# A routed two-layer kernel: expert slots of one size class per expert, of up to 512 tokens, in place of slots of 128 tokens

## The reference

```python
def attn(q, k, v, a):               # per batch (4) and head (8), 768 steps, 48 wide
    S = 0                           # complex 48 x 48
    for t in range(768):
        S = a[t][:, None] * S + outer(k[t], v[t])     # |a| clipped to 0.999
        y[t] = q[t] @ real(S)

def layer_a(x):                     # 3072 tokens
    logits = (x / |x|) @ (emb / |emb|).T / tau
    e = argmax(logits)
    return softmax(logits)[e] * (relu(x @ w1[e]) @ w2[e])

def layer_b(x):
    out = x
    for the tokens with x @ w_skip > 0:
        logits = x @ w_gate; e = argmax(logits)
        out = x + softmax(logits)[e] * (relu(x @ w1[e]) @ w2[e])
```

## Time and profile before

| what | us |
|---|---|
| median of 3 runs | 987.97 |
| lowest and highest | 987.32 and 994.53 |
| the profiled execution | 994.6 |
| its span in the profile | 993.0 |
| PE busy | 783.8 (79%) |
| DVE, ACT, POOL busy | 543.3, 454.0, 238.2 |

### The profile page before, as it was taken

The page is one execution under the profiler, slowest core; times in us unless marked ns, Lnnn a source line. Parts: engine busy times, 40 slices in busy tenths (PEclk is TensorE's granted clock), DMA queues, the critical chain, the costliest instruction groups (busy, mean ns, idle before and its releaser), DMA issues.

```text
span 993.0 us, 20046 instructions
## 1 busy us (share of the span) xinstructions
PE 783.8 (79%) x5035; PEld 680.6 (69%) x5036; DVE 543.3 (55%) x1395; ACT 454.0 (46%) x771; POOL 238.2 (24%) x267
## 2 busy tenths in 40 slices
PE   0598878968789896388989988898987179799991
PEld 0276757757677786277878877787877168788891
DVE  2556666767657654346555555656565226346630
ACT  6765526536436343064445444453642045344430
POOL 3307062170622411002211122222211113031120
PEclk9888688978959897599999999999999689899996
DMA  8361531815314171534222222324222216444200
GB/s 160 64 137 33 93 77 33 145 32 100 74 32 88 41 246 62 175 120 152 90 96 84 98 95 96 91 92 159 93 88 80 76 33 228 150 167 152 93 25 18
DMA packets 178428, 98.45 MB, mean 99 GB/s; under 512 B 148204, under 2 KB 167436, under 8 KB 178380
## 3 DMA queue, kind: packets, MB, share of 16 engines
q1 hardware_dynamic: 169612, 77.26, 28.7%
q0 software_dynamic: 8768, 20.64, 6.4%
HBM read 82.62 MB, written 21.85 MB: 105 GB/s over the span
## 4 chain that ended last, share of the span: by engine, by line
PE 57%; issue 16%; DVE 9%; ACT 6%; DVEq 4%; DMA 2%; ACTq 2%; SPq 1%; POOL 1%; POOLq 0%
PE bank L1510 10%; PE bank L1511 9%; PE bank L1512 9%; PE bank L1392 4%; PE bank L1381 3%; PE bank L1408 3%; PE bank L1370 3%; DVEq L1169 3%; PE bank L1409 3%; PE bank L1529 2%; PE bank L1357 2%; PE bank L1358 2%; PE bank L1354 1%; PE bank L1552 1%; PE bank L1419 1%
## 5 line engine op out<-in xcount | busy, mean ns | idle before, releaser
L1510 PE MATMUL bank<-w2h,hh 128*128 x344 | 125.7, 365 | 15.8 <-DVE w2l L1175 6.8
L1510 PE MATMUL bank<-w1h,xh 128*128 (+1 forms) x258 | 111.0, 430 | 15.2 <-DVE xl L1187 13.8
L1511 PE MATMUL bank<-w2l,hh 128*128 x344 | 121.8, 354 | 0.0
L1512 PE MATMUL bank<-w2h,hl 128*128 x344 | 121.4, 353 | 0.0
L1511 PE MATMUL bank<-w1l,xh 128*128 (+1 forms) x258 | 104.7, 406 | 0.0
L1512 PE MATMUL bank<-w1h,xl 128*128 (+1 forms) x258 | 104.5, 405 | 0.0
L831 ACT ACTIVATE hid<-bank 128x512 f32<-128x512 f32 x86 | 51.2, 598 | 107.5 <-PE bank L1512 105.9
L568 POOL DMA_INDIRECT rows_b<-yg,idx_b x27 | 26.9, 997 | 267.5 <-DVE yg L1274 267.5
L1510 PEld LDWEIGHTS bank<-w2h,hh 128*128 128x128 f32 x344 | 69.0, 201 | 22.3 <-issue 22.1
L867 ACT ACTIVATE hh<-bank 128x512 fp32r<-128x512 f32 x86 | 46.2, 589 | 71.2 <-PE bank L1529 71.0
L1305 DVE TENSOR_TENSOR hl<-bank,hh 128x512 fp32r<-128x512 f32 x86 | 55.3, 684 | 38.9 <-ACT hh L867 38.9
(11 more groups left out here) (211 smaller groups left out, 1838.6 us busy)
## 6 DMA issues: line engine op xcount, KB each, us to landing
raw<-in_moe_w SPq DMA_DIRECT2D x32, 1536.0 KB
xg<-rows_a POOLq DMA_DIRECT2D x27, 196.5 KB, 2.8
ar<-in_a_re SPq DMA_DIRECT2D x24, 192.0 KB, 3.6
...
```

The lines of the kernel that those rows point to most:

```text
L1510: t.matmul(out_, high[:, at], wh, start=c_ == 0, stop=False)
L1511: t.matmul(out_, high[:, at], wl, start=False, stop=False)
L1512: i = t.matmul(out_, low[:, at], wh, start=False, stop=c_ == n_ - 1)
```

## The change

Slots now hold up to 512 tokens of one expert (four tiles), so that an expert has one slot as long as it has no more than 512 tokens: `NS` falls from 31 to 13. A slot's length is one of 256, 320, 384, 448 or 512 columns, the smallest that holds its tokens. In the first product the weights are the stationary operand and the tokens move, which gives the hidden rows transposed, as the second product wants them; in A the second product is made in the same way, and its result (features by tokens) goes through products with the identity and gate_w at once, so that rows and B's logits come out of one set of products (`gate_w` holds the identity beside the gate columns, 137 wide). In B the second product stays as it was, tile by tile. PE has a copy of each product for each of the five lengths.

```diff
-NS = NT + E - 1
-NSP = 32
+NS = N // 512 + E - 1
+TJ = 4
+WIDE = TJ * P
+SIZES = (256, 320, 384, 448, 512)
```

```diff
+def row_out(b, c):
+    sp.wait_ge(s_y, B * c + b + 1)
+    sp.dma_start(x_a[bass.ds(b * S + c * P, P), :], ysb[:, b, :]).then_inc(s_x[b], 16)
-pool.wait_ge(s_idx, B * c + b + 1)
-g.indirect_dma_start(rows_a, bass.IndirectOffsetOnAxis(idx_a[:, b:b + 1], 0), ysb[:, b, :], None,
+pool.wait_ge(s_idx, 2 * c + b // 2 + 1)
+g.indirect_dma_start(list_of[0], bass.IndirectOffsetOnAxis(idx_a[:, b:b + 1], 0), token[:, c, b:b + 1], None,
+                     bounds_check=E * CAP - 1, oob_is_err=False).then_inc(s_put[b], 16)
...
+def members(s, par):
+    at = 0 if s == 0 else pool.value_load(tab[0:1, BASE + s:BASE + s + 1], min_val=0, max_val=E * CAP - WIDE)
+    g.dma_start(idx_g[:, par, :, 0:1 + m], list_of[m][bass.ds(at, WIDE), :].rearrange("(j p) w -> p j w", p=P),
+                allow_slow_non_contiguous=True).then_inc(s_list[m], 16)
+def gather(s, par):
+    pool.wait_ge(s_list[m], 16 * (s + 1))
+    for j in range(TJ):
+        g.indirect_dma_start(xg[:, par, j, 0:wide], None, rows, bass.IndirectOffsetOnAxis(idx_g[:, par, j, 0:1], 0),
+                             bounds_check=N - 1, oob_is_err=False).then_inc(s_xg[par][m], 16)
...
+if m == 0:
+    pool.wait_ge(s_side, s)
+else:
+    pool.wait_ge(s_yg[m], TJ * s)
+members(s + 1, par)
+pool.wait_ge(s_xT[m], KC * s)
+if m == 0:
+def scatter(s, par):
+    if m == 0:
+        pool.wait_ge(s_send, s + 1)
+        for j in range(TJ):
+            g.indirect_dma_start(list_of[1], bass.IndirectOffsetOnAxis(idx_b[:, par, j:j + 1], 0), pay[:, par, j, :], None,
+                                 bounds_check=E * CAP - 1, oob_is_err=False).then_inc(s_rows[par][m], 16)
+        pool.wait_ge(s_row, s + 1)
+    else:
+        pool.wait_ge(s_yg[m], TJ * (s + 1))
+    for j in range(TJ):
+        g.indirect_dma_start(out, bass.IndirectOffsetOnAxis(idx_o[:, par, j:j + 1], 0), yg[:, par, j, :], None,
+                             bounds_check=N - 1, oob_is_err=False).then_inc(s_rows[par][m], 16)
```

```diff
-for j in range(HP):
-    t.transpose(PY[:, j * DP:(j + 1) * DP], yT[:, b % 2, j * P:(j + 1) * P], ident[0:DP, 0:DP])
-for j in range(HP):
-    i = t.matmul(PY[:, HP * DP:HP * DP + E], yT[:, b % 2, j * P:(j + 1) * P], emb_T[:, j, :], start=j == 0, stop=j == HP - 1)
+for j in range(HP):
+    i = t.matmul(PY[:, j * DE:(j + 1) * DE], yT[:, b % 2, j * P:(j + 1) * P], aug[:, j, :], start=True, stop=True)
...
+    d.tensor_tensor(sum_a[:, :], sum_a[:, :], two_a[:, :], ALU.add).then_inc(s_sum, 1)
+dve.wait_ge(s_y, B * c + b + 2)
+d.reduce_max(mx_p[:, :], lg, AX.X).then_inc(s_mx, 1)
...
+d.tensor_tensor(oh_a[:, b:b + 2, :], each(ch_p[:, :]), pair(first_of[:, :]), ALU.is_equal).then_inc(s_oh, 1)
+d.tensor_tensor(at_f[:, :, :], PR.rearrange("p (t e) -> p t e", e=E), oh_a[:, b:b + 2, :], ALU.mult).then_inc(s_at, 1)
+d.tensor_tensor(two_a[:, :], oh_a[:, b, :], oh_a[:, b + 1, :], ALU.add).then_inc(s_two, 1)
+dve.wait_ge(s_at, k_ + 1)
+d.reduce_sum(at_s[:, :], at_f[:, :, :], AX.X).then_inc(s_at1, 1)
...
+d.tensor_scalar(idx_a[:, b:b + 2], at_s[:, :], -1.0, float(NOWHERE), ALU.mult, ALU.add).then_inc(s_idx, 1)
...
+    pe.wait_ge(s_sum, k_)
+pe.wait_ge(s_added, B * C if last else B * c + b + 3)
+two = PR.rearrange("p (t e) -> p t e", e=E)
+t.matmul(two, before_t[:, :], oh_a[:, b:b + 2, :], start=True, stop=False)
+t.matmul(two[:, 1, :], minus[:, :], oh_a[:, b, :], start=False, stop=False)
+t.matmul(two, minus[:, :], sum_a[:, :].unsqueeze(1).to_broadcast([P, 2, E]), start=False, stop=False)
+t.matmul(two, minus[:, :], starts[:, :].unsqueeze(1).to_broadcast([P, 2, E]), start=False, stop=True).then_inc(s_rank, 1)
```

In the layers the engines are written anew. ACT takes out each product and splits weights in pieces between them, DVE likewise:

```diff
+def up_out(s, size, run):
+    def parts(n):
+        for f in range(FC):
+            act.wait_ge(s_h[m], FC * s + f + 1)
+            a.activation(hh[:, f, 0:n], U[f % 3][:, 0:n], ACT.Relu).then_inc(s_hh[m], 1)
+            if f == 0:
+                act.wait_ge(s_w2in[m], run * 16)
+            high_part(w2h, raw2, HD, f).then_inc(s_w2h[m], 1)
+    sizes(size, parts)
...
+def parts(n):
+    for f in range(FC):
+        dve.wait_ge(s_hh[m], FC * s + f + 1)
+        d.scalar_tensor_tensor(out=hl[:, f, 0:n], in0=U[f % 3][:, 0:n], scalar=0.0, in1=hh[:, f, 0:n].bitcast(F32),
+                               op0=ALU.max, op1=ALU.subtract).then_inc(s_hl[m], 1)
+        dve.wait_ge(s_w2h[m], FC * s + f + 1)
+        low_part(w2l, w2h, raw2, HD, f).then_inc(s_w2l[m], 1)
+        if f == 2:
+            between()
+sizes(size, parts)
```

PE, with `n` columns of the slot, U three banks in turn, and `size` the number of tiles less 2:

```diff
+def rows_in(s, par, size):
+    pe.wait_ge(s_xg[par][m], (s - par) * 32 + 64)
+    if n_or_more(0, s, 1):
+        pe.wait_ge(s_hl[m], FC * s)
+    for tiles in (2, 3, 4):
+        with pe.If(size == tiles - 2):
+            for k_ in range(KC):
+                for j in range(tiles):
+                    i = t.transpose(U[k_][:, j * P:(j + 1) * P], xg[:, par, j, k_ * P:(k_ + 1) * P], ident[:, :])
+                i.then_inc(s_xT[m], 1)
+def up(s, n):
+    for f in range(FC):
+        if f >= 3:
+            pe.wait_ge(s_hl[m], FC * s + f - 2)
+        for k_ in range(KC):
+            wh = w1h[:, k_ * F + f * P:k_ * F + (f + 1) * P]
+            wl = w1l[:, k_ * F + f * P:k_ * F + (f + 1) * P]
+            t.matmul(U[f % 3][:, 0:n], wh, xh[:, k_, 0:n], start=k_ == 0, stop=False)
+            t.matmul(U[f % 3][:, 0:n], wl, xh[:, k_, 0:n], start=False, stop=False)
+            i = t.matmul(U[f % 3][:, 0:n], wh, xl[:, k_, 0:n], start=False, stop=k_ == KC - 1)
+        i.then_inc(s_h[m], 1)
+def down_a(s, n):
+    for d_ in range(KC):
+        if d_ == 2:
+            pe.wait_ge(s_yw, KC * s + 1)
+        for f in range(FC):
+            if d_ == 0:
+                pe.wait_ge(s_hl[m], FC * s + f + 1)
+                pe.wait_ge(s_w2l[m], FC * s + f + 1)
+            wh = w2h[:, f * HD + d_ * P:f * HD + (d_ + 1) * P]
+            wl = w2l[:, f * HD + d_ * P:f * HD + (d_ + 1) * P]
+            t.matmul(DN[d_ % 2][:, 0:n], wh, hh[:, f, 0:n], start=f == 0, stop=False)
+            t.matmul(DN[d_ % 2][:, 0:n], wl, hh[:, f, 0:n], start=False, stop=False)
+            i = t.matmul(DN[d_ % 2][:, 0:n], wh, hl[:, f, 0:n], start=False, stop=f == FC - 1)
+        i.then_inc(s_o[m], 1)
+def down_b(s, j, last):
+    if j >= 2:
+        pe.wait_ge(s_yg[m], TJ * s + j - 1)
+    elif n_or_more(0, s, 1):
+        pe.wait_ge(s_yg[m], TJ * s)
+    at = slice(j * P, (j + 1) * P)
+    for f in range(FC):
+        if j == 0:
+            pe.wait_ge(s_hl[m], FC * s + f + 1)
+            pe.wait_ge(s_w2l[m], FC * s + f + 1)
+        wh, wl = w2h[:, f * HD:(f + 1) * HD], w2l[:, f * HD:(f + 1) * HD]
+        t.matmul(DN[j % 2][:, 0:HD], hh[:, f, at], wh, start=f == 0, stop=False)
...
+with pe.If(size == tiles - 2):
+    for d_ in range(KC):
+        pe.wait_ge(s_yw, KC * s + d_ + 1)
+        for j in range(tiles):
+            if d_ == 0 and j == 3:
+                pe.wait_ge(s_yw, KC * s + 2)
+            i = t.matmul(R[j][:, d_ * GE:(d_ + 1) * GE], yw[:, d_, j * P:(j + 1) * P], gate_w[:, d_, :], start=True, stop=True)
+    i.then_inc(s_res, 1)
...
+def by_length(length, part):
+    for i, n in enumerate(SIZES):
+        with pe.If(length == i):
+            part(n)
...
+length, size = number(VAR, s, 4), number(TIL, s, 2)
+if more:
+    size_ = number(TIL, s + 1, 2)
+pe.wait_ge(s_w1l[m], s + 1)
+pe.wait_ge(s_xl[m], KC * s + KC)
+by_length(length, lambda n: up(s, n))
+if m == 0:
+    if n_or_more(0, s, 1):
+        rank_next(s - 1)
+    by_length(length, lambda n: down_a(s, n))
+else:
+    down_b(s, 0, False)
+if more:
+    with pe.If(used > s + 1):
+        rows_in(s + 1, 1 - par, size_)
+if m == 0:
+    results(s, size)
+else:
+    for tiles in (2, 3, 4):
+        with pe.If(size == tiles - 2):
+            for j in range(1, tiles):
+                down_b(s, j, j == tiles - 1)
...
+with pe.Fori(1, NS + 1, 2) as s:
+    with pe.If(used > s):
+        main(s, 1)
+        with pe.If(used > s + 1):
+            main(s + 1, 0)
```

More of the change, by code:

```diff
@@ L432, in _ @@
-            for run in range(3, E + 4):
-                load_w(run)
-            fill_ends(1)
-            for run in range(E + 4, 2 * E + 1):
-                load_w(run)
+                if e or m:
+                    tab, layer_, last = (tab_of[m], m, END + e - 1) if e else (tab_of[0], 0, USED)
+                    if e == 1:
+                        sp.wait_ge(s_tab, m + 1)
+                    done = sp.value_load(tab[0:1, last:last + 1], min_val=1, max_val=NS)
+                    sp.wait_ge(s_w1l[layer_], done)
@@ L439, in _ @@
+            for b in range(B):
+                row_out(b, C - 1)
+            for m in range(2):
+                for e in range(1 - m, E):
+                    load_w(m, e)
         @block.gpsimd
@@ L606, in _ @@
[L606 to L619 removed]
+                members(1, 1)
@@ new lines, in _, with step @@
+                gather(1, 1)
+                def step(s, par):
+                    if s + 1 < NS:
```

(55 more changed lines are left out.)

1129 lines of the change are left out of this document (496 added, 633 removed).

## The result

| us | kernel before | changed kernel |
|---|---|---|
| median | 988.83 (4 runs) | 1050.68 (4 runs) |
| lowest and highest | 987.32 and 994.53 | 1035.17 and 1056.16 |
| profiled execution, span | 994.6, 993.0 | 1048.38, 1046.8 |

The ratio of the times is 1.0525 (95% interval 1.0417 to 1.0633). The forecast was 886 with a range of 842 to 945, so it missed in size and in sign. The second rival, stalls at the skipped copies, gave 1047.

What follows compares the result with a forecast made beforehand. PE was taken to bound the kernel (busy 79% of the span). Terms -25 attention, -1.4 first change-over, -84 A, +7.3 second change-over, +1.1 B, 0 tail sum to -102: from median 988.0 to 886 us, range 842 to 945.

Steps and rivals of the forecast that it cites:

- second rival: Layers A and B: PE's jumps over skipped copies stall at 2.77 each, about 40% hidden, giving 1047 us; chance 7%.
- Attention, -25: Attention: later ranks spare PE's wait for oh_a (23), plus the router's partly hidden gain; -25 us, bounds 0 and -46.
- First change-over, 20: Attention to layer A: fill_ends goes, a list read, gathers and sends come; 20 us against 21.4, bounds 12 and 29.
- two last sends instead of one (+1.0): First change-over: one more send at the end adds 1.0 us.
- Layer A, 273: First expert layer: slots 255, cold clock 3, loop misses 15, total 273 us against 357.0; bounds 252 and 316.
- 255 + 3: Layer A without instruction misses: eight slots take 255 us, the slow clock at the start adds 3.
- I charge 2.8 plus one more such miss at each of three back edges: 15: Layer A: code-fetch stops of PE, priced by one 2.77 us jump and three loop jumps back, cost 15 us.
- Layer B, 176: Second expert layer: products, edges, cold start, late gathers and back edges take 176 us against 174.9; bounds 160 and 202.
- back edges partly hidden: 10: Layer B: stops at the loop's jumps back, partly hidden, cost 10 us.
- the 4 allowed: Layer B: gathers that come later than PE wants their rows cost 4 us.
- one such stop in seven long jumps: PE's jumps in the old trace: one of seven long ones stopped (2767 ns), so the skill page's rule holds only in part.
- rivals 1 and 3: Rival 1: everything hides, attention gives all, 839 us, 16%. Rival 3: slots' chain late, 4 more a slot, 950, 22%.

Runs made afterwards that it cites:

- e11: e7 with PE's rank products of a pair placed one tile earlier, in the tile right behind the pair; 880.69 us.
- e3: Changed kernel with wide lists: each list entry 64 bytes, written whole, in place of 4 in A and 8 in B; 1005.74 us.
- e8: Changed kernel with list entries still 4 bytes (8 in B) but spaced 64 bytes apart; 999.38 us.
- e7: Changed kernel with two copies of each part on PE, 64-byte list entries and PE's loop over slots written out; 868.02 us.
- e2: Changed kernel with one copy in A (448 columns, four tiles, no jump around large products) and two copies in B; 906.98 us.
- e1: Changed kernel with only the two copies of each part on PE that this input uses, in place of five; 912.97 us.
- e10: Changed kernel with all five copies, 64-byte list entries and PE's loop over slots written out; 976.05 us.

## Why the prediction was wrong

**Attention, -25, was right** (-23.2, with some 11 of chance between single executions). The wait of 38.8 fell to 1.8, and e11 shows the later ranks to be at least a good part of the gain.

**First change-over, 20, was wrong by 21.6.** The step that failed is "two last sends instead of one (+1.0)": the sends were charged for their issue, and the wait for them to land had no term. It measured 19.08, against 1.82 with wide lists, which shorten the stage by 16 (e3, e8). The list scatters send 128 writes each to eight short stretches of memory. The read of the list, priced at 3.2 after `dec`, took 4.1 to land: nearly right. The other 4 are PE's stop before A's first product, which five copies have (25.1 to 25.3 with wide lists) and fewer copies don't (21.0 to 22.2).

**Layer A, 273, was wrong by 70.8**, in one term. The products were right: 448 columns start 0.20 apart (forecast 0.203), and e7, in which none of PE's jumps inside A stops, has A in 254.0, against the sum without misses, 255 + 3. The term that failed is "I charge 2.8 plus one more such miss at each of three back edges: 15". (Its words don't give 15 either: three times 2.8 + 2.8 is 16.8, 2.8 and three times 2.8 are 11.2.) It was priced by counting jumps back, while the jumps past skipped copies, and straight code behind them, stopped as well. In A PE's gaps over 0.4 us sum to 85, against 11 in e7; on top of them comes the low clock behind the stops (0.88 against 0.99 and 1.00 in e7 and e2), which no term held: for the same products PE is busy for 264.2 in place of 244.5.

**Layer B, 176, was wrong by 59.5**, by the same term ("back edges partly hidden: 10"). The products with 256 columns start 0.12 apart:

```profile
799.22 0.28 PE L1585 MATMUL bank<-xh,w1h 128*128 128x256 f32 x1
799.34 0.28 PE L1586 MATMUL bank<-xh,w1l 128*128 128x256 f32 x1
799.46 0.28 PE L1587 MATMUL bank<-xl,w1h 128*128 128x256 f32 x1
```

so the value taken, 0.124, was right. With stalls gone B takes 168.8 to 175.8. There the gathers cost more than the 4 allowed: 3.6 to 4.2 at up to five slots in e7, 18.7.

**Second change-over, 35, and tail, 0**, measured 39.8 and -2.7: both inside their bounds (25 to 47, -5 to +5).

**The rivals.** The second had the place and almost the time (1047) and got 7%. By it the kernel was to be slower than before from 46 exposed misses on; there are 44 jumps over 1 us, of 3.3 on average, where it counted 112 of 2.77 with 40% hidden. That it came so near is in part luck: it had too many stops and left out others (in straight code), the clock behind a stop and the lists. It was discounted because "one such stop in seven long jumps" was read as a rate. But the seven stand behind the loop and pass one slot's short code each, and the 26 of L1614 stand at a loop whose body, about 400 instructions in A, stays at hand. The rows told of short code; the body of the changed kernel's loop is over eight times as long. The Trainium skill, page "Runtime: NRT & Kernel Launch", section "Instruction fetch mechanics", warns of just this, a taken branch out of what is at hand stops for a fetch. Its window of two 16 KiB pages, 512 instructions by its figures, does not fit these runs as it stands: the jumps back over about 1,100 instructions (e1, B) did not stop. The sentence of it that decides, fetch on a far jump, is borne out by e10.

The third rival (slots' chain late) had its effect only in B. Behind the failed term stands a chance set too low: 7% for a price that a row showed and that only its frequency made small. The range has a slip besides: it is said to take in rivals 1 and 3, but these gave 839 and 950, outside 842 to 945. It changes nothing here.
